# A matmul engine's first round of five tiles written out ahead of its loop

## The chip, the cores and the metric

The kernel runs on one core of one Trainium2 chip. The metric is the device time of one execution in microseconds (us), the median of several runs. Each engine of the core has a sequencer that reads its instructions in order and hands the work to the engine itself. For TensorE the profile shows both: PE are its matmuls, PEld its weight loads, and PEldq what the sequencer does itself (register arithmetic, waits on semaphores, loads of a register from SBUF, branches).

## The reference, cut to what matters

Three stages follow each other: a linear attention with a decay per head, a mixture of eight experts in which each of the 3072 tokens goes to one expert, and a gated feed-forward layer. The change lies in the second stage.

```python
# stage 2: N, D, E, F = 3072, 512, 8, 1024
e_idx = np.argmax(x @ w_gate + modality_bias[modality_id], axis=1)
for e in range(E):
    mask = e_idx == e
    h = np.maximum(x[mask] @ w1[e], 0.0)
    out[mask] = gate_w[mask, None] * (h @ w2[e])
# stage 3: x = (g(x @ w_in)) @ w_out, with d_ff = 2048
```

## The kernel before

All arithmetic is fp32 made of two parts: each operand is split into a high and a low part, and `split_products` (L2004) makes three matmuls of each product, on lines L2006, L2007 and L2008.

**Tiles.** The kernel sorts the tokens by expert into tiles of 128 rows. How many tiles there are depends on the data: 24 to 33. In this run there are 26. An expert tile i is one `expert_step` on TensorE (L2101): the expert's first product (`up`, 24 matmuls of 512 columns on `xT_hi`/`xT_lo`), four transposes that turn the rows of the next tile (`turn_rows`, L1865), then twice: half of the second product of the tile before (`down`, 12 matmuls on `hT_hi`/`hT_lo`) and four transposes of this tile's hidden rows (`turn_hidden`, L2045). That is 60 matmuls with a weight load each. Which expert and which half of the weight buffer a tile uses is read from a small table in SBUF into a register (`steering`, L526), so the weight addresses are computed from registers in every tile, whether it stands in a loop or not.

**The loop.** Tiles 0 to 2 are written out. Tiles 3 to 22 run in a loop of four rounds, five tiles in each (`READY_LOOPS` is 4, `XG_BUFS` is 5), because the buffer number goes round in five:

```python
with pe.Fori(0, READY_LOOPS) as it:
    round_of_tiles(it)
```

In a round `it` is a register, and the tile's number, the semaphore values that it waits for and the place in the table are computed from it. The other engines have their own loops over the same tiles and meet TensorE only at semaphores; the change leaves them alone.

**After the loop.** Tile 23 is written out, mixed with the transposes of the first finished rows (`turn_first`, L2123). Then `unsure_tiles` (L2158) holds the tiles that may or may not exist. It is a nest of `If`s, one inside the other, each with its `down_half` and the next tile's first half written out. When `used_tiles > i` is false, TensorE branches at L2161 over all the deeper levels to L2167, the second half of the last tile; then come the last `down` and the feed-forward stage, `pair` and `ff_down`, all straight code to the end of the program.

Of the kernel before, what the change touches and what calls it, by code (L numbers as in the profile page):

```python
# [60 lines left out]
READY_LOOPS = (TILES - FIRST_LOOPED) // XG_BUFS  # L61
# [159 lines left out]
def build(nc, qk, kv, modality, w_gate, mod_bias, w1, w2, w_quads, const, at, out):  # L221
    ctx = ExitStack()
    with ctx:
# [1626 lines left out]
        def _(pe):  # L1850
# [250 lines left out]
            def expert_step(i, buf, landed):  # L2101
                begin_tile(i, buf, landed)
                rank = steering(pe, i + (T_RANK - 1), 0, NE - 1)
                at_slot = pe.snap(slot_at(rank))
                for s in range(HALVES):
                    down_half(i, rank, at_slot, s)

            def round_of_tiles(it):
                for j in range(XG_BUFS):
                    i = it * XG_BUFS + (FIRST_LOOPED + j)  # L2110
                    nxt = FIRST_LOOPED + 1 + j
                    expert_step(i, nxt % XG_BUFS, DMA_INC * it + DMA_INC * (nxt // XG_BUFS + 1))
# [10 lines left out]
                    last = turn(ps_fT[j % 2][:, d, :], rows[:, d * P:(d + 1) * P], identity)  # L2123
                last.then_inc(fT_done, 1)

            with pe.Fori(0, READY_LOOPS) as it:
                round_of_tiles(it)

            landed_for = lambda i: DMA_INC * (i // XG_BUFS + 1)
# [201 lines left out]
```

## Time and profile before

| what | value |
|---|---|
| median of 3 runs | 926.84 us (926.23 to 927.27) |
| the profiled execution's own time | 927.58 us |
| its span, first to last instruction | 925.8 us |
| TensorE busy | 906.6 us, 98% of the span |
| mean granted TensorE clock | 0.996 of full speed |

The profiled execution is one more run than the three of the median. The 1.8 us between its time and its span lie outside the first and the last instruction. TensorE is the engine that is busy nearly all the time, so the time changes by what TensorE sits idle more or less, or by what it has more or less to do.

### The profile page before, as it was taken

The page shows a single profiled execution, that of the slowest core. Times are in us where ns is not written, and L with a number is a line of the kernel's source. Part 1 is how long each engine was busy: PE and PEld are TensorE (multiplying, and loading weights), DVE is VectorE, ACT ScalarE, POOL GpSimd, SP SyncE. Part 2 cuts the span into 40 slices and gives each one's busy share as a digit, 9 for nine tenths or more (in the row PEclk, how much of TensorE's full clock was granted, in tenths as well). Part 3 has the DMA queues.
Part 4 walks back from the last instruction along what each step waited for, and adds up shares of the span by engine and source line. Part 5 has one row for each costly group of instructions (what it writes and reads, how often), then busy time and mean ns, then how long its engine had stood idle before and what let it go on. Part 6 is the DMA issues. An engine that isn't in the chain of part 4 may idle for free.

```text
span 925.8 us, 18558 instructions
## 1 busy us (share of the span) xinstructions
PE 906.6 (98%) x6709; PEld 786.7 (85%) x6710; DVE 546.0 (59%) x861; ACT 393.8 (43%) x645; POOL 220.9 (24%) x231
## 2 busy tenths in 40 slices
PE   7998999999999999999999999999999999999998
PEld 5776788888888888887888999978899998889997
DVE  4679784555555542133645888544588854567663
ACT  1335424444444442233455554334555434454432
POOL 5537158532116814100120000232000021000003
PEclk9999999999999999999999999999999999999999
DMA  9999678998778866112575655677566567566554
GB/s 345 363 365 408 175 173 240 342 310 283 262 242 285 297 247 187 46 47 71 176 245 162 215 182 183 216 259 240 162 215 183 183 216 232 183 200 212 181 185 139
DMA packets 97216, 204.93 MB, mean 221 GB/s; under 512 B 7676, under 2 KB 50852, under 8 KB 97140
## 3 DMA queue, kind: packets, MB, share of 16 engines
q1 hardware_dynamic: 71056, 128.49, 43.0%
q10 hardware_dynamic: 19188, 55.64, 17.0%
q0 software_dynamic: 6896, 19.77, 7.0%
q8 instruction: 50, 0.82, 0.4%
q14 instruction: 26, 0.21, 0.1%
HBM read 148.00 MB, written 55.88 MB: 220 GB/s over the span
## 4 chain that ended last, share of the span: by engine, by line
PE 96%; issue 1%; DVE 1%; DMA 1%; POOL 1%; ACT 0%; POOLq 0%; SPq 0%; ACTq 0%
PE bank L2006 27%; PE bank L2008 27%; PE bank L2007 27%; PE bank L2045 2%; PE bank L1912 2%; PE bank L1883 2%; PE bank L1865 1%; PE bank L1921 1%; PE bank L1932 1%; PE bank L2123 1%; PE bank L1899 1%; DMA kv_in<-kv 1%; PE bank L1946 1%; DVE logits L1269 0%; PE bank L1953 0%
## 5 line engine op out<-in xcount | busy, mean ns | idle before, releaser
L2006 PE MATMUL bank<-ring,act_hi 128*128 128x256 f32 x672 | 190.5, 283 | 0.0
L2007 PE MATMUL bank<-ring,act_hi 128*128 128x256 f32 x672 | 190.2, 283 | 0.0
L2008 PE MATMUL bank<-ring,act_lo 128*128 128x256 f32 x672 | 190.1, 283 | 0.0
L866 ACT ACTIVATE act_hi<-act_f 128x1024 fp32r<-128x1024 f32 x84 | 88.9, 1058 | 117.6 <-PE bank L2008 117.6
L2006 PE MATMUL bank<-mix_hi,ring 128*128 128x512 f32 x336 | 131.6, 392 | 1.3 <-ACT h_sum L866 1.3
L2008 PE MATMUL bank<-mix_hi,ring 128*128 128x512 f32 x336 | 130.8, 389 | 0.0
L2007 PE MATMUL bank<-mix_lo,ring 128*128 128x512 f32 x336 | 130.8, 389 | 0.0
L2006 PEld LDWEIGHTS bank<-ring,act_hi 128*128 128x128 f32 x672 | 129.0, 192 | 0.5
L1719 DVE TENSOR_TENSOR act_lo<-act_f,act_hi 128x1024 fp32r<-128x1024 f32 x84 | 102.7, 1223 | 45.3 <-ACT act_hi L866 45.1
L2007 PEld LDWEIGHTS bank<-ring,act_hi 128*128 128x128 f32 x672 | 129.0, 192 | 0.1
L2008 PEld LDWEIGHTS bank<-ring,act_lo 128*128 128x128 f32 x672 | 129.0, 192 | 0.0
L813 POOL DMA_INDIRECT out<-f_out,token_idx x24 | 26.2, 1091 | 389.0 <-DVE f_out L1767 375.4
L1701 DVE TENSOR_TENSOR h_sum<-bank,h_sum 128x512 f32<-128x512 f32 x72 | 49.8, 692 | 105.3 <-PE bank L2008 101.5
L2006 PE MATMUL bank<-weights,hT_hi 128*128 (+1 forms) x208 | 86.9, 418 | 0.8 <-issue 0.8
L1287 DVE TENSOR_TENSOR hT_lo<-bank,hT_hi 128x512 fp32r<-128x512 f32 x52 | 35.8, 691 | 83.8 <-ACT hT_hi L866 81.2
L2006 PE MATMUL bank<-weights,xT_hi 128*128 (+1 forms) x208 | 83.6, 402 | 0.7 <-issue 0.5
L2008 PE MATMUL bank<-weights,hT_lo 128*128 (+1 forms) x208 | 82.4, 396 | 1.4 <-issue 1.4
L2007 PE MATMUL bank<-weights,hT_hi 128*128 (+1 forms) x208 | 81.9, 394 | 0.0
L2008 PE MATMUL bank<-weights,xT_lo 128*128 (+1 forms) x208 | 81.4, 391 | 0.0
L2007 PE MATMUL bank<-weights,xT_hi 128*128 (+1 forms) x208 | 81.1, 390 | 0.0
L2006 PEld LDWEIGHTS bank<-mix_hi,ring 128*128 128x128 f32 x336 | 63.1, 188 | 14.7 <-ACT h_sum L866 1.7
L2008 PEld LDWEIGHTS bank<-mix_hi,ring 128*128 128x128 f32 x336 | 63.1, 188 | 13.2
(246 smaller groups left out, 1516.3 us busy)
## 6 DMA issues: line engine op xcount, KB each, us to landing
ring<-w_parts SPq DMA_DIRECT2D x84, 512.0 KB
ring<-w_parts SPq DMA_DIRECT2D x24, 1024.0 KB
ring<-w_parts SPq DMA_DIRECT2D x24, 768.0 KB
w_parts<-part_hi ACTq DMA_DIRECT2D x16, 896.0 KB
qk_in<-qk SPq DMA_DIRECT2D x24, 512.0 KB, 8.7
raw<-w SPq DMA_DIRECT2D x24, 512.0 KB, 6.1
kv_in<-kv SPq DMA_DIRECT2D x20, 512.0 KB, 9.1
mix_in<-w_quads ACTq DMA_DIRECT2D x16, 512.0 KB
```

Source lines behind the costliest of these rows:

```text
L813: pool.indirect_dma_start(out=out, out_offset=bass.IndirectOffsetOnAxis(ap=token_idx[:, g % 2, j:j + 1], axis=0), in_=f_out[:, j, :], in_o ...
L866: copy = lambda dst, src: nc.scalar.activation(dst, src, ACT.Copy)
L1287: tt(hT_lo[:, part, :], ps_hT[s], hT_hi[:, part, :].bitcast(F32), ALU.subtract).then_inc(hT_split, 1)
L1701: tt(h_sum[:, at_, :], bank[k % 2][:, :], h_sum[:, at_, :], ALU.add).then_inc(h_ready, 1)
L1719: tt(act_lo[t % ACT_BUFS][:, :, :], operand(DOWN_ORDER[q], c), act_hi[t % ACT_BUFS][:, :, :].bitcast(F32), ALU.subtract).then_inc(act_spli ...
L1865: last = turn(ps_gT[:, d, :], xg[:, buf, d * P:(d + 1) * P], identity)
L1883: last = mm(ps_scores[par][keys, pair, queries], kT[rows, pair, keys], turned[rows, pair, queries], start=True, stop=True)
L1912: last = mm(x_place(h), values(t, h), masked[:, t % 2, (h % 2) * PAIRS + h // 2, :], start=(t % CHUNKS == 0 and h < 4), stop=(h >= 4), ski ...
L2006: mm(dst, hi, w_hi, start=first, stop=False, skip_group_check=skip)
L2007: mm(dst, hi, w_lo, start=False, stop=False, skip_group_check=skip)
L2008: return mm(dst, lo, w_hi, start=False, stop=last, skip_group_check=skip)
L2045: last = turn(ps_hT[s][:, a, :], hid[:, s * 4 + a, :], identity)
```

## The change

The first of the loop's four rounds is written out ahead of it, with the Python number 0 in place of the register. The loop then runs three rounds, 1 to 3. Nothing else is touched.

```diff
-            with pe.Fori(0, READY_LOOPS) as it:
+            round_of_tiles(0)
+            with pe.Fori(1, READY_LOOPS) as it:
                 round_of_tiles(it)
```

Three places in TensorE's program matter. First the place where tile 2 ends and the loop began. `MATMUL ... 128x512` is one matmul with its weight load, `ISA` and `REGISTER_ALU` are instructions of the sequencer. Before:

```order
L2045 MATMUL bank<-consts,hid 128x128 x8
L2126 UNCONDITIONAL_BRANCH
L2126 ISA
L526 TENSOR_LOAD steer
L526 ISA x2
L2012 REGISTER_ALU
L532 ISA
L2015 ISA
L2006 ISA
L2006 MATMUL bank<-weights,xT_hi 128x512
L2007 ISA
```

The same place of the changed program, where tile 3 now follows without a loop:

```order
L2045 MATMUL bank<-consts,hid 128x128 x8
L526 TENSOR_LOAD steer
L526 ISA x2
L2015 ISA
L2006 ISA
L2006 MATMUL bank<-weights,xT_hi 128x512
L2007 ISA
```

The loop's entry moved behind five written-out tiles, and each of these tiles has a few register instructions fewer than a tile in the loop. The loop itself is as long as before.

The third place is where the branch at L2161 lands, behind the nest of `If`s. The rows are those of before, from the last instruction of the nest; the changed program has the same rows with line numbers one higher.

```order
L2161 UNCONDITIONAL_BRANCH
L2167 REGISTER_ALU
L2167 ISA
L2028 ISA
L2006 ISA
L2006 MATMUL bank<-weights,hT_hi 128x512
L2007 ISA
L2007 MATMUL bank<-weights,hT_hi 128x512
L2008 MATMUL bank<-weights,hT_lo 128x512
```

Nothing moved within these rows. All of them, with everything behind the loop, stand further from the beginning of the program by the length of the five written-out tiles.

## Rows read from the trace of the kernel before

**Rows 1.** The page: busy time, share of the span, instructions.

```profile
PE 906.6 (98%) x6709; PEld 786.7 (85%) x6710; DVE 546.0 (59%) x861; ACT 393.8 (43%) x645; POOL 220.9 (24%) x231
```

**Rows 2.** Waits of PE from 140 to 441 us: total, times, longest.

```profile
PE bank L2008 <- issue: 1.4, 1, 1.4
PE bank L2006 <- issue: 0.8, 1, 0.8
```

**Rows 3.** First round's stretch: length, PE busy (matmuls), clock, DMA share, GB/s.

```profile
145.60:207.30 61.70, 61.70 (x303) 1.00 0.94 310
```

**Rows 4.** The loop's line L2126: duration in ns min/median/max, first and last start.

```profile
L2126 PEldq FUSED_REGOPS  x4: 68/68/68, 144.0 to 327.7; - x4
L2126 PEldq COMPARE_BRANCH  x4: 83/220/257, 204.1 to 389.0; - x4
```

**Rows 5.** DMA queues: page, then window 144 to 207 us.

```profile
q8 instruction: 50, 0.82, 0.4%
...
q8 instruction: 4, 0.07, 0.5%
```

**Rows 6.** All DMA queues in the third round, 268.9 to 330.6 us.

```profile
q10 hardware_dynamic: 4317, 14.42, 65.2%
q1 hardware_dynamic: 1088, 2.10, 11.9%
q0 software_dynamic: 448, 1.05, 6.6%
```

**Rows 7.** Window 490.8 to 904.6 us: PE, PEld (instructions) and other engines; then q8 there.

```profile
490.80:904.60 413.80, 412.51 (x2718) 379.81 (x2717) 275.06 (x322) 193.73 (x273) 27.63 (x32) 1.00 0.63 200
...
q8 instruction: 22, 0.36, 0.3%
```

**Rows 8.** The branches at L2165 and L2161, windows 400:410 and 420:430.

```profile
L2165 PEldq COMPARE_BRANCH  x1: 84/84/84, 405.7 to 405.7; - x1
...
L2161 PEldq COMPARE_BRANCH  x1: 3887/3887/3887, 426.3 to 426.3; - x1
```

**Rows 9.** q8 in windows 404.2:404.4, 427.8:427.9 and 433.5:433.6, in this order.

```profile
q8 instruction: 1, 0.02, 29.0%
...
q8 instruction: 1, 0.02, 59.9%
...
q8 instruction: 1, 0.02, 61.2%
```

**Rows 10.** Timeline of TensorE behind the branch: start, length in us; idle before in brackets.

```profile
429.23 0.60 PE L2045 MATMUL bank<-consts,hid 128*128 128x128 f32 x4
430.67 0.50 PE L2006 MATMUL bank<-weights,hT_hi 128*128 x1 [0.84 <-issue]
431.00 0.40 PE L2007 MATMUL bank<-weights,hT_hi 128*128 x1
...
433.90 0.48 PE L2006 MATMUL bank<-weights,hT_hi 128*128 x1
434.22 0.40 PE L2007 MATMUL bank<-weights,hT_hi 128*128 x1
435.97 0.50 PE L2008 MATMUL bank<-weights,hT_lo 128*128 x1 [1.35 <-issue]
```

**Rows 11.** Sequencer's register instructions: L2007 in 432:432.3, L2006 in 431.8:436.2.

```profile
L2007 PEldq FUSED_REGOPS  x1: 51/51/51, 432.1 to 432.1; - x1
...
L2006 PEldq FUSED_REGOPS  x2: 51/80/109, 431.9 to 436.0; - x2
```

**Rows 12.** Timeline of DVE and PE behind the second gap.

```profile
434.81 0.69 DVE L1287 TENSOR_TENSOR hT_lo<-bank,hT_hi 128x512 fp32r<-128x512 f32 x1 [3.63 <-ACT hT_hi L866]
...
436.08 1.22 DVE L1696 TENSOR_TENSOR mix_lo<-xT,mix_hi 128x1024 fp32r<-128x1024 f32 x1
...
441.09 0.39 PE L2006 MATMUL bank<-mix_hi,ring 128*128 128x512 f32 x1
```

**Rows 13.** Waits of PE from 440 to 926 us.

```profile
PE bank L2006 <- ACT h_sum L866: 1.3, 1, 1.3
```

## Prediction

> **What bounds the kernel.** I read the page first: TensorE is busy 98% of the span [rows 1], at full clock [rows 3], so only two things can move the time: TensorE's own work, or time in which it sits idle. The change leaves the matmuls as they are. So I asked the waits of PE where it is idle around the loop. From 140 to 441 us there are only two waits, both put down to "issue", which means that no semaphore held it [rows 2]. The windows of the four rounds say that neither is in the loop: the first is 61.7 us long and PE is busy for all of it [rows 3], and the other three are like it to 0.1 us. The timeline places both waits behind the branch at L2161, 0.84 us and 1.35 us [rows 10].
>
> **The loop's own cost.** What the change removes: one jump back (four rounds become three), and in five tiles the register arithmetic on `it`. The line of the loop shows the price on the sequencer: 257 or 220 ns for a branch that is taken, 83 ns for the one that leaves, 68 ns for the arithmetic behind it [rows 4]. That is about 0.3 us for one jump, and 26 register instructions fewer at 68 ns each at most, 1.8 us over 61.7 us. All of it is hidden: the sequencer runs ahead of the matmuls. How far ahead is seen at L2161, where it stops at 426.3 us and the matmuls handed over before keep PE busy until 429.83, that is 3.56 us [rows 8, 10]. A jump of 0.3 us against 3.5 us of work in hand costs nothing, and the round with a jump in it is as long as any other [rows 3]. If that cover were gone it would cost 0.3 us per jump. I count 0.0.
>
> **Where the instructions come from.** The only DMA queue that goes with TensorE's program is q8: 50 packets of 16.4 KB over the run [rows 5]. In the straight code from 490.8 to 904.6 us PE and PEld run 5435 instructions while q8 brings 22 packets [rows 7]; that is 247 for each packet, and with the sequencer's own instructions, which these rows leave out, some 253. So I take a packet for a block of 256 instructions (an estimate from these rows). The loop's first round fetches 4 packets [rows 5], and in a later one, as in all of them, q8 does not appear at all [rows 6]: the loop's 842 instructions are kept and a jump back finds them.
>
> The branch at L2161 at 426.3 us is different. The branch at L2165, which falls through, takes 84 ns, and this one 3887 ns [rows 8], and q8 brings one packet 1.5 us after it began [rows 9]: the place it lands on, some 1150 instructions ahead, was not there. TensorE sat idle for 0.84 us of these 3.9. Then there is a second gap of the same kind with no branch: the sequencer does a register instruction at 432.11 us and the next at 436.0 [rows 11], with a q8 packet again 1.4 us after the gap began [rows 9]. 432.16 to 435.96 is 3.80 us, the length of the first. I read it as the end of the block that was landed in: the next one had not been fetched ahead and was asked for only when the sequencer reached it. The trace agrees with the other fetches. Counted in the rows of the program, this gap lies 53 instructions behind the landing place at L2167, and the landing place lies 1684 behind the loop's end. So there are block ends 201 and 457 instructions behind the loop's end, 47 ahead of the branch at L2165 (405.7 us, place 248) and 78 ahead of the taken one (426.3 us, place 535) [rows 8]. The q8 packet at 404.3 us [rows 9], 1.4 us ahead of the branch at L2165, fits the first of them.
>
> **What the change adds, then, is a shift.** The five written-out tiles hold 815 instructions: 60 matmuls and 60 weight loads each, and 43 others (table loads, waits, weight addresses). 815 is 3 x 256 + 47. Everything behind the loop moves by 47 places within its block. The landing place was 53 instructions ahead of a block's end and will be 6 ahead of it: two at L2167, the one at L2028, the register instruction of L2006, one weight load and one matmul. This is the term of the sum, and it is worked out so:
>
> - The first gap stays: the branch misses as before, 3.9 us, of which PE feels 0.84.
> - The second gap begins at about 430.67 in place of 432.16, since the sixth instruction is the matmul that starts then [rows 10]. It lasts 3.80 us and ends at 434.47. With the register instruction at L2007 (0.05 us) and as much again to the start of the matmul, the second matmul starts near 434.55. Before, it started at 431.00 [rows 10]. That is 3.55 us late, since PE has one matmul in hand instead of some 2.5 us of work.
> - The old second gap goes: the matmul at 435.97 follows one of 434.22, where neighbours follow at 0.23 us (61.7 us less the transposes, over 240 matmuls in a round, is near 0.24). It cost 435.97 - 434.22 - 0.23 = 1.52 us.
> - Sum: 3.55 - 1.52 = +2.0 us.
>
> Nothing takes this back later. PE waits once more, 1.3 us for ACT's copy of a matmul result of its own [rows 13], and moves with it. Does the delay wake another wait? The last tile's transposes end at 433.90 and come 3.55 us later, while the work behind them comes only 2.0 later, so what hangs on them loses 1.5 us of slack. DVE's `hT_lo` ends at 435.50 [rows 12] and would end at 439.05; the 12 matmuls ahead of its user start at 433.90 + 3.55 and take 12 x 0.23 = 2.8 us, to 440.2. Slack 1.2 us, so no wait. `mix_lo` is ready at 437.30, then at 440.85, and is used from 441.09 on [rows 12], then from 443.1. In the written-out round the fetches run one block ahead, one each 19 us (256 of 842 instructions of 61.7 us), as in the loop's first round.
>
> So the profiled execution's 927.58 us would become 929.6. It is 0.74 us above the median of the three runs, which themselves spread over 1.04; against the median the forecast is 926.84 + 2.03 = 928.9 us.
>
> **A rule against this sum.** The back jump costs 220 to 257 ns and no packet [rows 4, 6]. The Trainium skill, page "Runtime: NRT & Kernel Launch", section "Instruction fetch mechanics", says that a taken branch whose target isn't in the current window of two pages forces a fetch, and that kernels prefer full unrolling for that reason. At L2161 the trace agrees (3887 ns). In the loop it doesn't: 842 instructions are over three blocks and are kept. The same section gives TensorE's instruction memory as 2048 instructions, in which the loop fits. By the rule each jump back would stall like L2161 and one less would gain; by the rows it gains nothing.
>
> **The rivals.**
> - *The next block comes a fixed time after the landing, whenever it is reached.* Then the second matmul starts at about 436.0 whatever its place: 436.0 - 431.0 - 1.5 = +3.5 us, 930.3 us. Against it: the two gaps are equally long, as two requests of one kind would be.
> - *The count is off by six or more*, so that the landing place falls at the head of a block. Then the next block's end is 250 instructions further, where PE has its full 3.56 us in hand and feels 0.84 like at L2161: 0.84 - 1.52 = -0.7 us, 926.2 us. For it: six instructions are a narrow margin, and branches without a row in the trace are counted by the program alone. Against it: the count gives 842 for a round and the trace's rounds agree.
> - *No effect:* the blocks go with the landing place and not with the program, and the second gap stays where it is: 926.8 us. Against it: the fetch at 404.3 us and the gap at 432.16 fit one fixed grid.
> - *Faster, by the jump back.* If a jump back stalled like L2161, one less would save 0.84 us where PE has work in hand (926.0 us) and all 3.9 us where it has none (922.9 us). It decides only if the jumps cost PE something, and PE is busy throughout [rows 3]: 0.3 us against 3.56.
>
> **How the numbers follow.** Forecast as summed 0.50, fixed time 0.12, count off 0.14, no effect 0.12, jump back 0.05, something unseen 0.07. The likeliest gives 928.9 with its own range 928.3 to 929.6 (gaps 0.2 to 0.3 us longer or shorter each, and the spread of the medians). The whole range reaches from the case of the miscount to the fixed time, 926.0 to 930.5, and leaves out under 2 in 10. A change of 0.2%, 1.85 us, is what this kernel's measurement can tell from none; that bound is 928.69, so about a quarter of the forecast's own weight falls within it. Slower: 0.75 x 0.50 + 0.12 + 0.03 = 0.52. Faster (under 924.99): 0.05. The same: 0.43.
>
> **What would show it.** In the changed kernel's trace: the waits of PE behind the skipped nest with one of 0.8 us at the first L2006 matmul and then one near 3.2 us at the next, at L2007, and none at L2008; the sequencer's gap right behind the landing; rounds of 61.6 to 61.7 us as before; about three q8 packets more in all; everything behind 441 us later by 2.0. A second gap that ends at the old 436.0 is the fixed time. A gap of 0.8 us near 460 us and none before is the miscount. A round shorter than 61.6 us would make me wrong about the loop.

## The result and the profile after

The changed kernel takes 931.33 us (median of 6 runs, 929.94 to 933.17); the kernel before, beside it, 926.54 (925.43 to 927.27). The ratio is 1.0053, with a 95% interval of 1.0040 to 1.0065: slower by 3.7 to 6.0 us. The forecast was 928.9 with a range to 930.5. The way was right and so was the place, the size was not: it is more than twice the +2.0 that was summed. A ratio in this document is not the quotient of the two medians beside it, and the two can differ by 0.1%.

The profiled execution has a span of 929.6 us and takes 931.5 us, like the median. First the waits of PE in it from 140 to 460 us, which answer to [rows 2]:

```profile
PE bank L2006 <- issue: 5.4, 1, 5.4
```

Two waits of 0.84 and 1.35 us have become one of 5.4 us. Next its timeline of PE behind the skipped nest, for [rows 10]; the number in brackets is the idle time ahead.

```profile
428.88 0.60 PE L2045 MATMUL bank<-consts,hid 128*128 128x128 f32 x4
434.91 0.59 PE L2006 MATMUL bank<-weights,hT_hi 128*128 x1 [5.44 <-issue]
435.29 0.63 PE L2007 MATMUL bank<-weights,hT_hi 128*128 x1
435.72 0.63 PE L2008 MATMUL bank<-weights,hT_lo 128*128 x1
436.15 0.63 PE L2006 MATMUL bank<-weights,hT_hi 128*128 x1
...
438.20 0.39 PE L2008 MATMUL bank<-weights,hT_lo 128*128 x1
438.43 0.39 PE L2006 MATMUL bank<-weights,hT_hi 128*128 x1
...
445.02 0.39 PE L2006 MATMUL bank<-mix_hi,ring 128*128 128x512 f32 x1
```

Two things are to be seen. The matmul that started at 430.67 in the kernel before starts at 434.91. And the eight matmuls from there to 438.20 follow each other at up to 0.43 us in place of 0.23. The reason for that stands in the windows of the same kernel (length, PE busy with count, granted clock, DMA share, GB/s), 435 to 438 us:

```profile
435.00:438.00 3.00, 3.00 (x8) 0.50 0.03 5
```

The granted clock is half, 1.2 in place of 2.4 GHz, and 8 matmuls run in it. In as long a window of the kernel before, 431 to 434 us at full clock, there are 13 of these matmuls and 4 short transposes. The Trainium skill, page "TensorE: Matmul & The Clock Gate", Part 1, says that this clock is gated by how busy TensorE has been of late; the trace agrees, PE had been idle for 5.2 us when the granted clock fell at 434.7 us. The sequencer's own rows, of the branch (now L2162), its landing place (L2168), and the register instructions of L2006 and L2007 between 429.3 and 434.95 us, for [rows 8, 11]:

```profile
L2162 PEldq COMPARE_BRANCH  x1: 3397/3397/3397, 425.9 to 425.9; - x1
...
L2168 PEldq ALU_OP  x1: 42/42/42, 429.4 to 429.4; - x1
...
L2006 PEldq FUSED_REGOPS  x1: 114/114/114, 429.7 to 429.7; - x1
...
L2007 PEldq FUSED_REGOPS  x1: 51/51/51, 434.9 to 434.9; - x1
```

The second gap begins right behind the landing, as forecast, but it is 5.1 us long in place of 3.8. The loop is as it was, its line and its first round's stretch for [rows 3, 4]:

```profile
L2127 PEldq COMPARE_BRANCH  x3: 83/220/256, 265.4 to 388.7; - x3
...
145.30:207.00 61.70, 61.70 (x304) 1.00 0.89 310
```

and q8 brings 54 packets, four more than in [rows 5], where about three had been forecast (from its page):

```profile
q8 instruction: 54, 0.88, 0.4%
```

From the start of the far branch to the first matmul of the feed-forward stage it is 445.02 - 425.92 = 19.10 us; in the kernel before 441.09 - 426.27 = 14.82 [rows 12]. So 4.3 us of the 4.8 lie in this stretch. The rest of the difference of medians is within the interval.

Ahead of the branch nothing changed. From the matmul that starts behind the last wait ahead of the loop (137.47 us in the kernel before, 137.11 in the changed one) to the start of the far branch, a stretch that holds all four rounds, it is 288.80 us and 288.81 us.

### The profile page after: what moved, and what is told of

It is laid out like the page before. It is cut to its first block, busy times and chain, and to the rows that moved or that the text cites. A ratio compares the mean times of both kernels' runs of the same rounds, so it can differ in the third digit from the quotient of the medians.

```text
span 929.6 us, 18531 instructions
## 1 busy us (share of the span) xinstructions
PE 906.7 (98%) x6709; PEld 786.9 (85%) x6710; DVE 546.2 (59%) x861; ACT 393.8 (42%) x645; POOL 219.9 (24%) x231
## 4 chain that ended last, share of the span: by engine, by line
PE 93%; DVE 3%; issue 2%; DMA 1%; POOL 1%; ACT 0%; POOLq 0%; SPq 0%; DVEq 0%; ACTq 0%
PE bank L2006 27%; PE bank L2008 27%; PE bank L2007 26%; PE bank L1912 2%; PE bank L2045 2%; PE bank L1883 2%; PE bank L1921 1%; PE bank L1865 1%; PE bank L1932 1%; PE bank L2123 1%; PE bank L1899 1%; DMA kv_in<-kv 1%; PE bank L1946 1%; DVE lane_hot L1524 0%; DVE hT_lo L1287 0%
## 5 line engine op out<-in xcount | busy, mean ns | idle before, releaser
L2006 PE MATMUL bank<-ring,act_hi 128*128 128x256 f32 x672 | 190.5, 283 | 0.0
L2007 PE MATMUL bank<-ring,act_hi 128*128 128x256 f32 x672 | 190.2, 283 | 0.0
L2006 PE MATMUL bank<-mix_hi,ring 128*128 128x512 f32 x336 | 131.6, 392 | 1.3 <-ACT h_sum L866 1.3
L2007 PE MATMUL bank<-mix_lo,ring 128*128 128x512 f32 x336 | 130.8, 389 | 0.0
L2006 PEld LDWEIGHTS bank<-ring,act_hi 128*128 128x128 f32 x672 | 129.0, 192 | 0.5
L2007 PEld LDWEIGHTS bank<-ring,act_hi 128*128 128x128 f32 x672 | 129.0, 192 | 0.1
L2006 PE MATMUL bank<-weights,hT_hi 128*128 (+1 forms) x208 | 86.6, 417 | 5.4 <-issue 5.4
L2006 PE MATMUL bank<-weights,xT_hi 128*128 (+1 forms) x208 | 83.6, 402 | 0.8 <-DVE xT_lo L1276 0.6
L2007 PE MATMUL bank<-weights,hT_hi 128*128 (+1 forms) x208 | 81.9, 394 | 0.0
L2007 PE MATMUL bank<-weights,xT_hi 128*128 (+1 forms) x208 | 81.1, 390 | 0.0
L2006 PEld LDWEIGHTS bank<-mix_hi,ring 128*128 128x128 f32 x336 | 63.1, 188 | 14.5 <-ACT h_sum L866 1.7
L866 ACT ACTIVATE hT_hi<-bank 128x512 fp32r<-128x512 f32 x52 | 30.9, 598 | 103.4 <-PE bank L2045 100.8
```

What stands on the lines that cost most here:

```text
L866: copy = lambda dst, src: nc.scalar.activation(dst, src, ACT.Copy)
L2006: mm(dst, hi, w_hi, start=first, stop=False, skip_group_check=skip)
L2007: mm(dst, hi, w_lo, start=False, stop=False, skip_group_check=skip)
```

## The experiments

Theory A: the time comes from where the landing place of the far branch falls in its block of 256 instructions, and from nothing else. Rival B: the written-out round, or one round less in the loop, costs it. To move the landing place and nothing else, instructions are put into the deepest level of the nest of `If`s, which never runs for this data:

```diff
+            def never_run(n):
+                for _ in range(n // 2):
+                    turn(ps_fT[0][:, 0, :], hid[:, 0, :], identity)
+                ...
             def unsure_tiles(i, rank, at_slot):
                 if i < MAX_TILES:
                     with pe.If(used_tiles > i):
+                        if i == MAX_TILES - 1:
+                            never_run(48)
                         ...
```

The number is 48, 60, 32, 46 and 16 in the kernel before, and 208 and 12 in the changed one. Each run's ratio is to the kernel before on the same chip, whose medians were 925.3 to 925.6 us. A transpose is two instructions, a weight load and a matmul; the `...` stand for lines left out here, which matter for an odd number only.

**48 in the kernel before.** 

> The kernel before (loop of four rounds, nothing written out), with 24 transposes (48 instructions) put into the deepest level of the nest of Ifs, which never runs for this data; the program behind the nest moves by 48 places. Theory A (the whole loss is where the landing place of the far branch falls in its block of 256): the same as the changed kernel, 931.3 us, +4.8 over before, with one idle stretch of PE of about 5.4 us at the first matmul behind the landing and then about 3.4 us at half clock. Rival B (the written-out round itself, or one round less in the loop, costs the time): 926.5 us, no change.

Measured 931.01 us, ratio 1.0058 (1.0040 to 1.0076). The loop has all its four rounds here, and the loss is that of the changed kernel. Its timeline:

```profile
435.64 0.80 PE L2006 MATMUL bank<-weights,hT_hi 128*128 x1 [5.68 <-issue]
436.23 0.63 PE L2007 MATMUL bank<-weights,hT_hi 128*128 x1
```

**208 in the changed kernel.** 

> The changed kernel with 104 transposes (208 instructions) in the level that never runs, so that the shift is a whole number of blocks (48 + 208 = 256). Theory A: 926.5 us as before, gaps of 0.84 and 1.35 us at the old places, no half clock. Rival B: 931.3 us as the changed kernel.

Measured 924.38 us, ratio 1.0002 (0.9989 to 1.0015). The written-out round is in it and the time is that of before; the two waits are back at their old places (its timeline):

```profile
432.45 0.50 PE L2006 MATMUL bank<-weights,hT_hi 128*128 x1 [0.70 <-issue]
437.25 0.40 PE L2008 MATMUL bank<-weights,hT_lo 128*128 x1 [0.85 <-issue]
```

These two settle A against B: the loss comes without the change, and the change comes without the loss.

**60 in the kernel before.** 

> The kernel before with 60 instructions that never run: the landing place falls a few instructions behind the head of a block, some 249 ahead of its end. Theory A with the next block arriving a fixed 5.6 us after the landing: it is there long before it is needed, the second gap is gone, only 0.84 us of idle are left, -1.5 us, 925.0 us. Theory A with the next block asked for only when it is reached: a gap of 3.8 us on the sequencer about 20 us behind the landing, of which PE feels up to 0.8 us, 925.8 us. Rival B: 926.5 us.

Measured 923.44 us, ratio 0.9987 (0.9975 to 0.9998). Its wait of PE from 140 to 926 us, the only one, and below it its q8 in the windows 425.9:426.1 and 431.4:431.6:

```profile
PE bank L2006 <- issue: 0.8, 1, 0.8
...
q8 instruction: 1, 0.02, 30.0%
...
q8 instruction: 1, 0.02, 30.8%
```

The second gap is gone and none came in its place. The second packet decides between the two readings of the gap: it came 5.5 us after the first although the sequencer had some 170 instructions of the landing block still ahead (counted in its rows). So it isn't asked for when the end of the block is reached. It comes by itself, a nearly fixed time after the first.

**32 in the kernel before.** 

> The kernel before with 32 instructions that never run: the landing place is 21 ahead of a block's end and six matmuls go out before it. Fixed time (the second gap ends 5.6 us after the landing): the seventh matmul starts 3.7 us late, less the old 1.5, +2.1 us, 928.7 us, and 930.1 us if the clock falls to half for 3.4 us as in the changed kernel. Asked for when reached (3.8 us from the end of the block): +1.2 us, 927.7 us. Rival B: 926.5 us.

Measured 929.23 us, ratio 1.0044 (1.0027 to 1.0062). Its timeline has both the late packet and the half clock:

```profile
429.17 0.50 PE L2006 MATMUL bank<-weights,hT_hi 128*128 x1 [0.53 <-issue]
434.37 0.50 PE L2006 MATMUL bank<-weights,hT_hi 128*128 x1 [3.55 <-issue]
...
437.27 0.63 PE L2007 MATMUL bank<-weights,hT_hi 128*128 x1
```

**46 in the kernel before.** 

> The kernel before with 46 instructions that never run: the landing place is 7 ahead of a block's end, so one matmul goes out before it, which is the layout that the prediction took for the changed kernel (it turned out one place further). If missing that one place mattered, this is 928.5 or so; theory A (the next block 5.5 us after the first, and then half clock) says that it does not: an idle stretch of 0.8 and one of about 4.7 us, half clock for 3.4 us behind it, +0.5% over before, as the changed kernel.

Measured 932.04 us, ratio 1.0071 (1.0056 to 1.0086). One matmul goes out ahead of the gap, as I had thought for the changed kernel, and it makes no difference that the runs can tell: its interval and that of 48 overlap (its timeline):

```profile
429.94 0.49 PE L2006 MATMUL bank<-weights,hT_hi 128*128 x1 [0.83 <-issue]
435.00 0.79 PE L2007 MATMUL bank<-weights,hT_hi 128*128 x1 [4.57 <-issue]
```

**12 in the changed kernel.** 

> The changed kernel with 12 instructions that never run: written-out first round as it is, landing place at the head of a block. Theory A: only the first gap is left, as in the run pad60, 0.1 to 0.2% under before. Rival (the written-out round costs something of its own that a placement hides): slower than that by its price; above before if the price is over 1.3 us.

Measured 924.61 us, ratio 0.9988 (0.9976 to 1.0001). The landing place has just passed the end of a block, and the changed kernel is as fast as the kernel before with 60.

**The nest cut short.**

```diff
-                if i < MAX_TILES:
+                if i < TILES + 3:
                     with pe.If(used_tiles > i):
```

> The kernel before with the nest of Ifs cut to the levels that this data reaches (it leaves out the handling of more than 27 tiles). The branch then goes over some 165 instructions and lands in a block that is there already. Theory A: no long branch, both gaps gone, 0.84 + 1.52 us, -0.25% against before. Rival (a taken branch forward stalls whatever its distance): 3.9 us on the sequencer and 0.84 us of idle as before.

Measured 923.0 us, ratio 0.9970 (0.9957 to 0.9983). The branch line of this kernel:

```profile
L2161 PEldq COMPARE_BRANCH  x2: 73/144/216, 414.5 to 426.8; - x2
```

The taken branch costs 216 ns here, as much as a jump back of the loop. From 120 to 926 us no wait put down to "issue" is left. So a taken branch forward is not expensive in itself. What differs is the distance, some 165 instructions in place of some 1150, and with it whether the landing place had been fetched; the run does not tell these two apart. The loop's jump back, over 842 instructions that had run before, cost 220 to 257 ns [rows 4], which speaks for the second.

**The last round written out in place of the first.**

```diff
-            with pe.Fori(0, READY_LOOPS) as it:
+            with pe.Fori(0, READY_LOOPS - 1) as it:
                 round_of_tiles(it)
+            round_of_tiles(READY_LOOPS - 1)
```

> The last of the four rounds written out behind the loop in place of the first ahead of it; the code behind it moves by the same 815 or 816 places. Theory A: as the changed kernel, +0.5% over before, with the same 5.4 us and half clock. Rival (it is the first round, while the other engines load and split weights, that suffers): 926.5 us.

Measured 931.47 us, ratio 1.0062 (1.0048 to 1.0077), with one wait of 5.3 us at the same matmul. So it does not matter that it was the first round.

**16 in the kernel before.** 

> The kernel before with 16 instructions that never run: the landing place is 37 ahead of a block's end; 12 matmuls go out before the second gap, and the four transposes and two matmuls that went out too in the kernel before, 0.8 us of work, don't. It asks for the price of the idle time apart from that of the clock. If the clock stays up: the second idle stretch 2.2 us in place of 1.35, +0.8 us, +0.1%. If it falls to half as in the runs with 3.5 us of idle and more: +0.8 and another 1.4 to 1.6 us, +0.25%.

Measured 926.78 us, ratio 1.0022 (1.0009 to 1.0035), single runs from 924.85 to 930.35. In the profiled run the second idle stretch is 2.05 us and the clock falls behind it (its timeline):

```profile
431.34 0.50 PE L2006 MATMUL bank<-weights,hT_hi 128*128 x1 [0.78 <-issue]
436.39 0.92 PE L2045 MATMUL bank<-consts,hid 128*128 128x128 f32 x4 [2.05 <-issue]
437.54 0.63 PE L2007 MATMUL bank<-weights,hT_hi 128*128 x1
```

The interval reaches from +0.1%, the idle time alone, to +0.35%; the forecast with the clock was +0.25%. But the clock falls in some of the executions only: the profiled one, with 3.4 us at half clock, has a mean granted clock of 0.998, and the one of 926.78 us has 1.000.

**The changed kernel with the nest cut short.** 

> The changed kernel with the nest of Ifs cut in the same way as in the run nest_cut (it leaves out the handling of more than 27 tiles): the written-out round alone, with no far branch whose landing it could shift. Theory A: the same as nest_cut, -0.3% against before, no gap around the loop. Rival (the written-out round has a price or a gain of its own): above or below nest_cut by it, 0.3 us if the jump back had cost what it takes on the sequencer.

Measured 923.52 us, ratio 0.9984 (0.9974 to 0.9994), against 0.9970 (0.9957 to 0.9983) for the cut nest with the loop whole. These were measured on different chips. The ratios differ by 0.14%, and by their intervals alone a price of the written-out round of up to 0.3% isn't excluded; a gain from it isn't seen. The traces bound it closer. The stretch of 288.80 us from the last wait ahead of the loop to the far branch in the kernel before is 288.73 to 288.82 us in all twelve kernels profiled, with the first round, the last or none written out, so a written-out round costs or gains less than 0.1 us. From there to the feed-forward stage it is 12.08 us in both kernels with the nest cut short. The taken branch took 363 ns in this one, where it was 216.

## Why the prediction was right and wrong

**The loop's own cost, 0.0: right.** The first round's stretch is 61.7 us with PE busy throughout, in the loop and written out. The changed kernel with 208 is even with before. The far branch took 3397 to 3897 ns in the ten profiles that have it, the loop's jump back 220 to 262. The Trainium skill, page "Runtime: NRT & Kernel Launch", section "Instruction fetch mechanics", says that a taken branch to a target outside the current window of two pages forces a fetch. The trace agrees at the far branch and disagrees in the loop, whose 842 instructions are over three blocks of 256: its jump back brings no packet [rows 4, 6].

**The shift of the landing place: right to one instruction.** The last instruction that got out ahead of the gap was the first weight load, at 429.82 us; I had counted the first matmul too. The runs show no difference between one matmul out ahead of the gap and none: 46 and 48 are alike within their intervals.

**"It lasts 3.80 us and ends at 434.47": this step failed.** I took the second packet for one that is asked for when the sequencer reaches the end of the block, because the two gaps of the kernel before happened to be equally long. The packets say otherwise. The second comes 5.7 us after the first packet of the landing in the kernel before (427.8 and 433.6), 5.6 in the changed one (426.9 and 432.5), 6.1 with 32 (426.1 and 432.2) and 5.5 with 60 (426.0 and 431.5), with the end of the block 53, 5, 21 and some 249 instructions behind the landing. The second gap ended 5.8 us after the landing in the kernel before and 5.6 in the changed one. That the two gaps of the kernel before were alike, 3.89 and 3.80 us, was chance: the second is what was left of those 5.8 us when the sequencer reached the end of the block. The fixed time was the first rival, at 0.12, and the equal length was the only thing that spoke against it. Measured from the start of the branch, the second matmul comes at 9.37 us in the changed kernel and at 4.73 before, 4.6 us late in place of 3.55; less the old 1.52 that is +3.1, not +2.0.

**A term was missing: the clock.** After 5.4 us of idle PE runs at half the granted clock until 438.1, and the eight matmuls up to 438.20 take 3.29 us, where the same eight took 1.95 in the kernel before (430.67 to 432.62). From the first matmul behind the landing to the feed-forward stage it is 10.11 us; in the kernel before 10.42 - 1.52 = 8.90. So the clock took about 1.2 us. 3.1 + 1.2 = 4.3 us is what the stretch shows. I had asked what PE's idle time costs and not what it does to PE afterwards. The clock fell behind or within the longest idle stretch there in the six profiles in which it was 2.05 to 5.68 us long, and in none of the other six, in which it was 1.35 us at most; that it is the idle time that brings it down is read from this alone. What it takes varies. In the profiled execution with 48 PE runs at half clock from 435.64 to 441.7 us, and from its far branch to the feed-forward stage it is 20.83 us against 19.10 in the changed kernel, 1.5 of it behind the first matmul. Its window from 435.7 to 440 us:

```profile
435.70:440.00 4.30, 4.30 (x10) 0.50 0.01 4
```

**Nothing takes it back later: right.** PE's only wait behind 440 us is the same 1.3 us for ACT, and from the first matmul of the feed-forward stage to the end it is 484.6 us in the changed kernel and 484.7 before. The shift has nothing to do with this wait: it is 0.5 us in the profile with 16 and absent in the other nine. Neither `hT_lo` nor `mix_lo` was waited for.

**The measured time lies above the range** because the range ended with the first rival alone, 930.3, and the clock comes on top of it: 926.84 + 4.3 = 931.1.

**A version faster than both** is the kernel before with 60 instructions that never run, faster than the kernel before by 0.1% (0.0 to 0.25%). It handles all numbers of tiles. The cut nest is faster by 0.3% but leaves out cases.

## What to carry to other kernels

Writing a loop's round out, or any edit of straight code, moves all that is behind it within the blocks in which instructions are fetched. In these traces that cost nothing in the loop and in straight code, but behind the far branch the time depended on how many instructions lay between the landing place and the end of its block. After such an edit, look for "issue" waits behind far branches and shift the landing place with code that never runs. Placing rarely needed code where it need not be jumped over may help too; no run here tried that, only leaving it out. When an edit makes TensorE idle for some microseconds, add the price of its clock to the sum: here about 1.2 us behind 5.4 us of idle.

## What the runs showed that I had not expected

In the ten profiles that have it, the far branch brings a block 1.0 to 1.6 us after it starts, TensorE's sequencer goes on after 3.4 to 3.9 us, and the next block follows 5.4 to 6.1 us after the first, whether it is needed or not. That is also 2.9 to 3.5 us after the sequencer goes on; the traces do not tell which of the two starts it. A landing 5 to 7 instructions ahead of a block's end cost 0.5 to 0.7% over the kernel before, one 21 ahead 0.4%, and the same branch landing at a block's head cost 0.4 to 0.8 us of idle time. In the profiled run with 16 the clock fell behind idle stretches of 0.78 and 2.05 us; in that of the kernel before it stayed at full behind 0.84 and 1.35. As the clock did not fall in every execution with 16, these are no bounds.
